# A delta-rule scan with two feed-forward stages: a Gram matrix of k taken against a narrow copy of its transposes, and the inverse's two fp16 halves taken earlier

## The reference, cut to what matters

```
k_n = k / (norm(k) + 1e-6)
for t in range(768):                                  # for each batch and head
    y[t]  = q[t] @ state
    state = state + beta[t] * outer(k_n[t], v[t] - k_n[t] @ state)
x = y as (3072, 384)
x = max(0.01 h, h) @ w_out,  h = x @ w_in             # 384 -> 2048 -> 384
out = x;  where x @ w_skip > 0:  e = argmax(x @ w_gate)
          out = x + prob[e] * (relu(x @ w1[e]) @ w2[e])     # 8 experts, 384 -> 1024 -> 384
```

## Time and profile before

| | |
|---|---|
| Time, median of 3 runs | 931.82 us (930.31 to 933.48) |
| The profiled execution's own time | 934.12 us |
| Its span, first to last instruction | 932.4 us |
| Mean granted clock of TensorE | 0.955 of 2.4 GHz |
| PE busy | 801.2 us, 86% |
| PE weight loads | 648.3 us, 70% |
| DVE busy | 650.3 us, 70% |
| ACT busy | 500.6 us, 54% |
| POOL busy | 415.9 us, 45% |

### The profile page before, as it was taken

The page is one execution under the profiler, slowest core; times in us unless marked ns, Lnnn a source line. Parts: engine busy times, 40 slices in busy tenths (PEclk is TensorE's granted clock), DMA queues, the critical chain, the costliest instruction groups (busy, mean ns, idle before and its releaser), DMA issues.

```text
span 932.4 us, 27901 instructions
## 1 busy us (share of the span) xinstructions
PE 801.2 (86%) x10858; PEld 648.3 (70%) x10859; DVE 650.3 (70%) x1303; ACT 500.6 (54%) x1099; POOL 415.9 (45%) x500
## 2 busy tenths in 40 slices
PE   0314769999999999999999999999956899999986
PEld 0313648888787878787878788887735677788864
DVE  5378877887878888888888877865666825533382
ACT  4435545767576766666766666555454514412261
POOL 4314242626363635454454524343314646644463
PEclk9975698999999999999999999999986999999998
DMA  9782844676766766747575475420645833611100
GB/s 240 131 213 44 144 76 82 122 119 129 117 131 115 122 127 122 130 93 151 92 144 105 91 133 100 84 58 19 198 142 198 303 119 122 223 51 51 36 22 16
DMA packets 309830, 109.97 MB, mean 118 GB/s; under 512 B 284930, under 2 KB 301364, under 8 KB 309344
## 3 DMA queue, kind: packets, MB, share of 16 engines
q1 hardware_dynamic: 304000, 94.63, 48.9%
q0 software_dynamic: 3232, 7.64, 2.4%
q10 hardware_dynamic: 2496, 6.29, 1.9%
HBM read 60.39 MB, written 20.46 MB: 87 GB/s over the span
## 4 chain that ended last, share of the span: by engine, by line
PE 61%; DMA 11%; DVE 9%; SPq 7%; issue 4%; ACT 4%; POOL 3%; DVEq 0%; POOLq 0%; ACTq 0%
PE b_acc L681 16%; PE b_h L668 15%; PE b_ch L606 9%; PE b_acc L807 8%; PE b_h L791 7%; SPq L453 4%; DMA natq<-x_dram,id_in 3%; PE b_gr L572 3%; DMA operands<-t_dram 3%; DMA t_dram<-inv 3%; PE b_ch L572 2%; DMA natq<-in_q_dram 1%; DVE inv L1234 1%; ACT inv L826 1%; DVE inv L1228 1%
## 5 line engine op out<-in xcount | busy, mean ns | idle before, releaser
L1612 POOL TENSOR_TENSOR stage<-stage 128x256 f16<-128x256 f32 x192 | 142.4, 742 | 266.7 <-ACT stage L826 266.0
L668 PE MATMUL b_h<-stage,wt 128*128 128x256 f16 x1728 | 221.6, 274 | 5.2 <-DVE stage L1298 3.2
L681 PE MATMUL b_acc<-wt,stage 128*128 128x384 f16 x1152 | 219.4, 327 | 2.4 <-POOL stage L1612 0.4
L668 PEld LDWEIGHTS b_h<-stage,wt 128*128 128x128 f16 x1728 | 159.6, 98 | 26.1 <-DVE stage L1298 6.1
L681 PEld LDWEIGHTS b_acc<-wt,stage 128*128 128x128 f16 x1152 | 106.2, 98 | 59.7 <-POOL stage L1612 6.9
L826 ACT ACTIVATE stage<-stage 128x256 f16<-128x256 f32 x192 | 80.0, 416 | 98.7 <-DVE stage L1298 97.7
L1298 DVE SCALAR_TENSOR_TENSOR stage<-b_h,stage 128x256 f32<-128x256 f32 x192 | 80.6, 420 | 69.3 <-ACT stage L937 69.1
L807 PE MATMUL b_acc<-wt,operands 128*128 128x384 f16 x576 | 101.6, 326 | 7.0 <-DVE operands L1530 7.0
L791 PEld LDWEIGHTS b_h<-y,wt 128*128 128x128 f16 x1728 | 100.3, 99 | 8.3 <-issue 6.3
L791 PE MATMUL b_h<-y,wt 128*128 128x128 f16 x1728 | 102.9, 222 | 3.2 <-DVE y L1161 2.9
L572 PE MATMUL b_gr<-operands 128*128 128x128 f16 x576 | 44.6, 233 | 53.1 <-DMA operands<-operands 20.6
(11 more groups left out here) (174 smaller groups left out, 1269.8 us busy)
## 6 DMA issues: line engine op xcount, KB each, us to landing
operands<-in_moe_w_dram SPq DMA_DIRECT2D x16, 1536.0 KB, 7.5
a_sys<-a_dram SPq DMA_DIRECT2D x24, 256.0 KB, 4.3
natq<-in_q_dram SPq DMA_DIRECT2D x24, 192.0 KB, 3.9
raw_v<-in_v_dram SPq DMA_DIRECT2D x24, 192.0 KB, 4.1
stage<-y SPq DMA_DIRECT2D x96, 48.0 KB, 2.1
x_dram<-stage SPq DMA_DIRECT2D x24, 192.0 KB, 2.8
out_dram<-stage SPq DMA_DIRECT2D x24, 192.0 KB, 3.2
natk<-in_k_dram SPq DMA_DIRECT2D x22, 192.0 KB, 4.0
```

What stands on the lines that cost most here:

```text
L668: mm = pe.matmul(b_h[f % 2][:, 0:GT], wt[0][:, a, d * FF + f * P:d * FF + (f + 1) * P], xT[:, g % 2, b, d, :], start=(i == 0), stop=(i == ...
L681: mm = pe.matmul(b_acc[w][:, 0:DM], g16[:, f % 4, a, w * P:(w + 1) * P], wt[1][:, b, f * DM:(f + 1) * DM], start=(f == 0 and (a, b) == PAR ...
L1612: pool.tensor_tensor(g16[:, f % 4, LO, :], g32[:, f % 4, :], g16[:, f % 4, HI, :], ALU.subtract).then_inc(g_lo, 1)
```

## The change

The moving operand of `gram_a` becomes `kTc`, 64 columns wide: for each unit only the diagonal block of either half, without the zero blocks. Its products and `ga` are half as wide. `kTc` is filled by `compact_k(g)`, two DMAs in SBUF that SP issues right behind `turn_k(g)` (64 partitions, 32 pieces of 128 bytes each); for group 0 it is filled by one copy on ACT and one on DVE. `compact_k` first waits for the transposes to land and for the last `gram_a` of the group before. Constants of the routing that lay in the second half of `ga` move to `kc`. And at step 12 (13 in turn 0) ACT takes `inverse_high` ahead of `p_high`, and DVE takes `inverse_low` ahead of `gate_x_low` and `leaky`.

```diff
@@ tiles
-        ga = sb("ga", [P, NU, P])
+        kc = sb("kc", [P, 2 * NU * C], F16)
+        kTc = kc[:].rearrange("p (l u i) -> p l u i", l=2, u=NU)
+        ga = sb("ga", [P, NU, C])
-        spare = ga[:].rearrange("p u i -> p (u i)")[:, 1024:2048]
+        spare = kc[:].bitcast(F32)
@@ sync
+            def compact_k(g):
+                sp.wait_ge(k_turned[g % 2], 32 * (g // 2) + 32)
+                sp.wait_ge(ga_done, B * g)
+                for x in range(2):
+                    h = slice(C * x, C * x + C)
+                    sp.dma_start(kTc[h].rearrange("p l u i -> p (l u) i"),
+                                 kT[g % 2][h, :, :, h].rearrange("p l u i -> p (l u) i")).then_inc(kc_loaded, 16)
@@ blocks_out
-                    sp.dma_start(a_w[b], ga[BLK * b:BLK * b + BLK, :, BLK * b:BLK * b + BLK]).then_inc(a_stored, 16)
+                    sp.dma_start(a_w[b], ga[BLK * b:BLK * b + BLK, :, BLK * (b % 2):BLK * (b % 2) + BLK]
+                                 ).then_inc(a_stored, 16)
@@ sync, turn(g)
                 if is_group(g + 2):
                     turn_k(g + 2)
+                    compact_k(g + 2)
@@ sync, prologue
             turn_k(1)
+            compact_k(1)
             load_k(2)
             load_q(1)
             blocks_out(0)
@@ tensor, gram
+                n = rhs.shape[3]
-                        mm = pe.matmul(b_gram[st % 2][:, p * P:(p + 1) * P], kT[g % 2][:, a, u, :], rhs[:, b, u, :],
+                        mm = pe.matmul(b_gram[st % 2][:, p * n:(p + 1) * n], kT[g % 2][:, a, u, :], rhs[:, b, u, :],
@@ tensor, gram_a
+                if g:
+                    pe.wait_ge(kc_loaded, 32 * g)
+                else:
+                    pe.wait_ge(kc_copied, 2)
-                gram(kT[g % 2], g, st).then_inc(ga_done, 1)
+                gram(kTc, g, st).then_inc(ga_done, 1)
@@ scalar, gram_out
-                    i = copy(ga[:, u, :], b_gram[st % 2][:, p * P:(p + 1) * P], nb256[:, g * NU + u:g * NU + u + 1])
+                    i = copy(ga[:, u, :], b_gram[st % 2][:, p * C:(p + 1) * C], nb256[:, g * NU + u:g * NU + u + 1])
@@ scalar, turn(g)
+                    if nxt and f == (12 if g else 13):
+                        inverse_high(g + 1)
                     if nxt and 12 <= f < 15:
                         p_high(g + 1, f - 11)
-                    if nxt and f == (12 if g else 13):
-                        inverse_high(g + 1)
@@ scalar, prologue
             split_w_in(0)
+            act.wait_ge(k_turned[0], 32)
+            copy(kTc[0:C], kT[0][0:C, :, :, 0:C]).then_inc(kc_copied, 1)
             for x in range(2):
                 kn_high(1, x)
@@ vector, turn(g)
                     if inv and mid > at:
                         inverse(n, at, mid)
+                    if nxt and f == (12 if g else 13):
+                        inverse_low(g + 1)
                     if gate and f in (13, 14):
                         gate_x_low(g - 1, f - 13)
...
                     if nxt and f == 4:
                         a21_low(g + 1)
-                    if nxt and f == (12 if g else 13):
-                        inverse_low(g + 1)
@@ vector, prologue
+            dve.wait_ge(k_turned[0], 32)
+            dve.tensor_copy(kTc[C:P], kT[0][C:P, :, :, C:P]).then_inc(kc_copied, 1)
             split_w_in(0)
@@ gpsimd, constants
                     pool.wait_ge(a21_ready, G)
+                    pool.wait_ge(ga_done, B * G)
```

More of the change, by code:

```diff
@@ L210, in build @@
         q_ready = sem("q_ready")
+        kc_copied = sem("kc_copied")
+        kc_loaded = sem("kc_loaded")
         k_turned = [sem("k_turned0"), sem("k_turned1")]
@@ L873, in a21_high @@
                 for h, c in ((slice(0, BLK), slice(BLK, 2 * BLK)), (slice(C, C + BLK), slice(C + BLK, P))):
-                    i = copy(a21[h, HI, :, c], ga[h, :, c])
+                    i = copy(a21[h, HI, :, c], ga[h, :, BLK:2 * BLK])
                 i.then_inc(a21_hi, 1)
@@ L1194, in a21_low @@
                 for h, c in ((slice(0, BLK), slice(BLK, 2 * BLK)), (slice(C, C + BLK), slice(C + BLK, P))):
-                    i = dve.tensor_tensor(a21[h, LO, :, c], ga[h, :, c], a21[h, HI, :, c], ALU.subtract)
+                    i = dve.tensor_tensor(a21[h, LO, :, c], ga[h, :, BLK:2 * BLK], a21[h, HI, :, c], ALU.subtract)
                 i.then_inc(a21_ready, 1)
```

## The result

The changed kernel takes 923.82 us, the median of 5 runs (921.53 to 924.88), beside 931.82 for the kernel before in 5 runs of its own (930.31 to 934.34): ratio 0.9905, with a 95% interval of 0.9888 to 0.9922. It is 8.0 us faster, by the ratio 7.2 to 10.4. Forecast were 15, so the sign was right and the size near half. The profiled execution took 924.88 us, 9.2 less than the one profiled before.

A forecast was written before the change was run, and what follows sets the result against it. PE was taken to bound the steady turns. Narrow Gram -11.5, halves -5.0, turn 0 -2.0 and prologue +3.5 sum to -15.0 us: 919 us for the profiled execution, median 917, range 908 to 930.

The forecast's parts named there:

- in the steady turns PE sets the pace: Steady turns: PE is busy 47.4 of 48.5 us and waits only for the inverse over DRAM, 6.3 us in 8 waits.
- the term of -11.5: Turns 1 to 9: the narrow gram_a saves 1.28 us a turn on PE, 11.5 us in all (10.6 to 13.2).
- The price of the narrow matmuls: gram_a's 48 matmuls of 64 columns: 29.1 ns each, 26.7 ns saved on each, 1.28 us a turn.
- Rival 4: gram_a: narrow matmuls don't shorten because the weight load sets the distance; 928 us, chance 0.02.
- The halves: Inverse taken 1.7 us sooner at step 12, worth 5 us in the turns; 2.7 us sooner in turn 0.
- Rival 2: Steady turns: DVE becomes the bound, half of the 1.28 us goes through, waits stay at half; 924 us, chance 0.12.
- The compaction at 0: Steady turns: copies land 5.3 us after the transposes, 1.4 us before gram_a, hidden under PE's steps 3 to 5; price 0.
- Rival 3: Steady turns: compact_k lands after gram_a is due, 2.2 us late a turn, 20 us in all; 937 us, chance 0.12.
- The prologue: Before the first inverse: new copies and queue waits shift SP's loads 5.0 us later; +3.5 us, range -2 to +6.
- the three cases of part 4: Prologue stall: follows items ahead, 5.0 to 6 us later; ends when it ends, nothing to 2; gone, 2 gained.
- Turn 0: Turn 0: inverse 2.7 us sooner inside PE's wait of 4.51, copies in SP's queue cost 0.7; -2.0 us in all.
- the signs named: Profile after: 0.35 us per 12 matmuls, turns of 46.5 us, few waits; against it, turns above 47.5 with DVE waits.

The follow-up runs named there:

- halves with T first: Kernel before with both inverse halves sooner and, in SP's queue, inverse_out ahead of blocks_back, load_k behind inverse_back: 918.67 us, ratio 0.9855.
- narrow Gram alone: Changed kernel with inverse_high and inverse_low back at their old places: 932.03 us, ratio 0.9987.
- the halves alone: Kernel before with only the calls of inverse_high and inverse_low moved: 923.5 us, ratio 0.9883.
- the run without the compaction: Changed kernel without compact_k and its waits, groups 1 to 11 multiplied with group 0's kTc: 919.36 us, one run.
- the wait alone: Changed kernel where SP still waits for k_turned and ga_done but issues none of compact_k's DMAs: 921.52 us, one run.
- the late compaction: Changed kernel with compact_k(1) moved behind blocks_out(0) in SP's prologue: 922.06 us, ratio 0.9865.
- DVE's copies: Changed kernel with SP's compact_k gone; DVE copies kTc in two instructions at step 5 of each turn, group 1's in the prologue: 946.89 us, ratio 1.0131.
- the kernel with `x_low` sooner: Changed kernel with DVE taking x_low ahead of the inverse's share of steps 8 and 9: 938.61 us, ratio 1.0075.

## Why the prediction was half right

**The step that failed** is the first one, "in the steady turns PE sets the pace", and with it the term of -11.5: that PE's 1.28 us a turn come through whole. PE's own work was 47.6 us a turn (halves with T first: 380.7 without its waits, by 8), the loop through `tT` 48.5 or more. The longer one was the loop, by 0.9 us. The 6.3 us of waits in the earlier trace rows were read as an extra on top of PE's pace; they were the mark of the loop that set it. The narrow Gram alone therefore gave the 0.59 us by which it shortens that loop, 4.2 us in seven turns, and not 1.28. And PE's saving didn't get through the loop's first part because of a second limit close by: `x_low` was ready 0.30 us before PE needed it, and beyond that and the little that DVE gains PE only waits.

**The price of the narrow matmuls** was right: 29 ns per matmul by the distance of starts, 1.28 us a turn by the rows of 26.17 and 27.45 above. PE's busy time is no clean measure of it, 7.6 less with the narrow Gram alone and 10.1 with both parts. Rival 4 is out, and with it the Trainium skill's pair rule weighed there.

**The halves** were right in size: 1.64 us of 1.7 in the loop. Their worth was put at -5.0 in the turns and -2.7 in turn 0; alone they gave 5.9 in turns 2 to 9 and 1.0 up to turn 0's end. Of the 5.9 the waits explain 2.5, and PE's busy time, 2.0 less for the same 5617 matmuls, another 2; the rest is in gaps too short for the view of waits. The busy time falls because the modelled ends of matmuls cover short waits. Late in the turn at 287.49 `up`'s piece at 328.30 takes 1.27 us to the next start, and the gate's at 330.56 takes 0.47; with the halves alone those at 325.88 and 327.84 take 0.98 and 0.25. So 0.5 us of short waits behind step 12 are gone in that turn, with the same matmuls. That the waits for `tT` would end was wrong: 2.3 us stayed, where 1 was forecast, and waits of other kinds for 6.7 came.

**Rival 2** (DVE becomes the bound, half of the 1.28 comes through, 924) came nearest, by time and by mechanism: 0.59 of 1.28 came through, and what held the rest was DVE's `x_low`. But it named DVE alone. `x_low` is 2.8 of 9.0 us of waits in the changed kernel; the rest is the round trip and SP's queue. That its 924 is within 0.2 of the measured time is luck in part: its terms for the turns, turn 0 and the prologue were -9, -2 and +3.5, measured were -10.8, -0.4 and +2.4.

**The compaction at 0** in the steady turns: right in the result, and in six of eight turns in the reason. It was to land 5.3 us after the transposes (measured 4.6 to 6.1) and leave 1.4 us to spare. The transposes' own landing was read from one turn, 11.5 us into it, and scatters: 8.5 to 13.3 after. In the turn shown they landed only at 346.84, 12.8 into the turn, and in two of eight turns `gram_a` was late, by 0.9 at most. The worst landing of one DMA, 8.4 us, is as long as the upper bound, but it fell in the prologue. Rival 3, 2.2 us a turn, is far off. The copies still do harm: `y_out` and `turn_q` come later, by 0.7 and 1.7 us in the median. In turns 2 to 9 that hid under the loop, as the run without the compaction shows; it costs 3.6 us once the loop is short.
The Trainium skill (SBUF — State Buffer, The DMA setup-cost knee) gives a fit of 2 us and bytes over 436 GB/s; for 256 KB that would be an estimate of 2.6 us. The trace doesn't agree, with 3.2 at best and 4.4 in the median for 2048 pieces of 128 bytes.

**The prologue**: +3.5 forecast, +2.39 measured (53.11 to 55.50). `turn_k(1)` moved by 0.84 us (29.28 to 30.12), not by 1.9. The rows of SP's queue after:

```profile
35.72 1.69 SPq L421 DMA_DIRECT2D kc<-operands  x2
37.45 5.63 SPq L400 DMA_DIRECT2D natk<-in_k_dram  x2
43.13 3.24 SPq L406 DMA_DIRECT2D natq<-in_q_dram  x2
46.41 2.39 SPq L442 DMA_DIRECT2D a_dram<-ga  x4
```

The stall of 7 us in the earlier trace rows sat in `blocks_out(0)` and ended at 46.24; now it sits in the loads ahead, and ends at 46.4. The items in which it sits in the queues of the wait alone, and of the late compaction:

```profile
37.70 8.66 SPq L405 DMA_DIRECT2D natq<-in_q_dram  x2
```

```profile
38.26 8.95 SPq L442 DMA_DIRECT2D a_dram<-ga  x4
```

end at 46.4 and 47.2. It ends when it ends, whichever item stands in it: one of the three cases of part 4, and not the one I took. But that case was priced at "nothing to 2", and `blocks_out(0)` stands behind the stall now and pays its own 2.39 us after it. What the queue waits for there stays open. `gram_a(1)` waited for its copy too, in the timeline of PE:

```profile
44.91 0.80 PE L589 MATMUL b_gr<-kc,operands 128*128 128x64 f16 x12 [14.67 <-DMA kc<-operands]
```

14.67 us that cost nothing that the rows show: the next `scan_u` hangs on the inverse.

**Turn 0**: -2.0 forecast against the prologue. `inverse_out` gained 1.6, not 2.7 (issued at 129.00, before 128.18, with the first inverse 2.4 later), and the way back grew by 1.2 (12.3 us to `scan_u` at 141.30, before 11.1 to 139.30), so turn 0 gave back 0.4. The longer way back comes with the halves too: 12.1 to 12.4 us in the three kernels that have them sooner in SP's old order and no copies. PE's timeline:

```profile
109.83 0.90 PE L677 MATMUL b_tr<-ident,stage 128*128 128x128 f32 x3 [3.50 <-DMA stage<-y]
...
141.30 0.83 PE L627 MATMUL b_ch<-z,operands 128*128 128x48 f16 x24 [3.87 <-DMA operands<-t_dram]
```

`compact_k(2)` now stands with `load_k(3)` ahead of `y_out` (issued at 105.44, before 98.33), and PE waits 3.50 us for it there and 2.29 at 113.66. With the wait alone `y_out` is issued 2.7 us sooner, counted from `scan_u`, and `inverse_out` has its full gain; so the 1.5 us lost are the copies' own. That they reach `inverse_out` through PE's wait for `y_out` is argued, not shown. That "DVE and PE have nothing in reserve" was right; 0.7 for it was too little. The 2.7 for the halves was right (2.9 with them alone). Turn 1 made it good: it took 48.7 us, before 50.7, and at 190 us the two kernels are level.

**The sum, term by term**, forecast and measured between the profiled executions: prologue +3.5, +2.4; turn 0 -2.0, -0.4; turns 1 to 9 -16.5, -10.8 (2.1 up to 190 us and 8.7 behind); the rest 0, -0.5. That is -15.0 and -9.3.

Of the signs named, the price of the 12 matmuls came. Four did not come: turns of 46.5 us, waits for `tT` near 1 us, a wait under 2 us at the end of turn 0 (it was 3.87), and no wait on `kc`. The one against came: turns above 47.5 us (47.7 in the mean) with DVE's waits ahead of the first layer's matmuls.

Open is what puts `x_low` at 27 us into each turn on DVE, beside the links of the inverse and the waits for ACT; the hand-overs there were not taken apart. DVE's waits for ACT's `hidden` pieces (`stage L958` after, `stage L937` before) fell from 39.6 to 19.7 us in the eight turns, so it does wait less.

## What to carry to other kernels

A wait that comes back each turn, however short, can be the mark of a loop that sets the pace: measure that loop from end to end, in several turns, before you count an engine's saving in full. A length that is the same to 0.05 us each time is only a hint (with the narrow Gram alone, and with DVE's copies, it was as constant at another length). That a loop is the bound shows when PE waits at its end in every turn and an edit that shortens the loop alone shortens the turn; then a saving counts by what it takes off the loop. Look, too, for what is ready only just in time: `x_low` was 0.30 us ahead of need, and it took most of a saving of 1.28. Where several limits lie within 1 us in 48, an edit is worth its distance to the next one: change the longest first, then try the others again on top of it.

## What the runs showed that was not expected

- 2.2 us more work on DVE in a turn made the turn 3.4 longer; part of that is the clock, which stood at its lower level (0.50 from 324 to 326 us) behind PE's wait of 2.66.
- A wait of PE of 1.84 and one of 1.87 us were followed by such a fall too, one of 1.85 in the kernel with `x_low` sooner was not (granted clock 1.00 over its eight turns).
- The same 64x2048 f16 copy took 0.69 us on DVE (0.91 and 1.29 inside the turns) and 1.89 on ACT. Timelines of the changed kernel's prologue, DVE and then ACT:

```profile
23.09 0.69 DVE L1484 COPY kc<-operands 64x2048 f16<-64x2048 f16 x1 [0.73 <-DMA operands<-operands]
...
24.04 1.89 ACT L847 ACTIVATE kc<-operands 64x2048 f16<-64x2048 f16 x1
```

- Two DMAs more in a queue made its neighbours slower to issue, not only later: `y_out`'s eight issues took 6.65 us in the median of turns 2 to 9 after (5.25 to 7.61), 6.14 before (5.62 to 6.36) and 5.76 with the wait alone (5.32 to 6.07).
- The stall of SP's queue in the prologue keeps its end (45.7 to 47.2 us in all fourteen profiled kernels), whatever is queued.
